# A fused attention, Fourier-mixing and gated-conv kernel: the value windows of its local attention loaded in runs of four heads, eight transfers a unit

## The chip, the cores and the metric

The kernel runs on one core of one Trainium2 chip. The metric is device microseconds of one launch, here the median of three runs. The profile is that of one further execution; its span runs from its first to its last instruction.

## What is computed

Three stages for a batch of 4, sequence length 576, 8 heads of 64 (512 features). All inputs are fp32.

```
x  = pooled attention (q, k, v averaged over groups of 4 tokens, output repeated 4 times)
   + local attention  (mask: |i - j| < 4)
u  = x + real(fft(fft(x, axis=seq), axis=features))
y  = u + relu(layernorm(u) @ w_ch1) @ w_ch2          (512 -> 2048 -> 512)
out = (sigmoid(causal_conv5(y)) * (y @ w_val)) @ w_out
```

Both attentions are `softmax(q k^T / 8) v`, with 1e-9 added to the sum of the exponentials.

## The kernel before, in words

The program is written engine by engine, with semaphores. It has five steps: a first one that does the attention and the mixing of batch 0 (and prepares the weights), a loop of three steps, each of which does the MLP, conv and output of one batch and, between their matmuls, the attention and mixing of the next, and a last step with the MLP, conv and output of batch 3.

**Units.** The attention of a batch is cut into 13 units: 8 pooled ones, one for each head, and NT = 5 local ones (t = 0 to 4). A local unit holds four windows of 32 queries each, for all 8 heads: its scores tile is 128 x 304, with rows = 4 windows x 32 queries and columns = 8 heads x 38 keys. A unit goes through these stages, in different iterations of the program's slots:
- scores (L384 lays the mask, L389 adds q k^T, 16 matmuls of 32 x 76: a pair of heads for one window), 
- subtraction of the row maximum (DVE, L878 and L884), exponential (ACT, L665), the division for local units (DVE, L892 to L898), 
- transposition (PE, L417: four of 128 x 76, one for each pair of heads) and its copy to `probT` (ACT, L673),
- AV (L446 adds the pooled result, L452 the local one: 16 matmuls of 32 x 128, again a pair of heads for one window), and the copy to `x` (ACT, L683 to L686).

On PE the order of the first step is, in each slot: transposition of unit u-2, scores of unit u, AV of unit u-2. So the scores of local unit 2 stand ahead of the AV of unit 0. In the loop the scores of local units stand two slots of the MLP apart, at slots 9, 11, 13, 15 and 17, and the AV three slots behind its scores.

**Loads of a local unit.** `ql`, `kl` and `vl` have two buffers each. SP issues all of these loads, in order, from `attend_loads` and `window` (L336 to L350): first q and k of units 0 and 1, then v of units 0 and 1, then for t = 2, 3, 4 the q and k of unit t (after the scores of unit t-2 have been computed) and the v of unit t (after the AV of unit t-2). For q there is one transfer (L343), for k there are two, one for each head of a pair (L345), and for v four (L349):

```
for s in range(2):
    for j in range(2):
        sp.dma_start(vl[i][LK * j:LK * j + LK, 2 * s:2 * s + 2, :, j, :],
                     v_win[b, t, 32 * s:32 * s + LK, :, j:H:2, 0:D]).then_inc(ld_v[i], 16)
```

Each of them moves 38 rows (keys) x 2 windows x 4 heads (every second one) x 64 floats. In `v_win` the last dimension has 65 floats, so each head's 64 floats are a run of 256 bytes of their own: 304 runs in a transfer, 76 KB. In `vl` rows 0 to 37 hold the keys of the even heads and rows 38 to 75 those of the odd heads, each with zeros in the other head's columns; POOL writes these zeros once (L1239).

**Weights in the first step.** From the slot of local unit 2 on, ACT and DVE also split the weights w1 and w2 into two fp16 parts, in 16 chunks: DVE takes the maximum (L981, `weight_max`), ACT scales (L753, `weight_high`), DVE takes the remainder (L1007, `weight_low`), ACT copies back (L758). The second half of them starts after `weight_scale(1)` (L993 to L1001), which DVE reaches after the folds (`fold`, L925 to L941, with POOL's part at L1204). ACT's queue also issues the loads of w1 and w2, 1 MB each (L736, L739).

Of the kernel before, what the change touches and what calls it, by code (L numbers as in the profile page):

```python
# [19 lines left out]
B, H, N, D = 4, 8, 576, 64  # L20
# [9 lines left out]
LQ, LK = 32, 32 + 2 * BAND  # L30
# [10 lines left out]
WCH = KD * F // WCW  # L41
# [9 lines left out]
def fused_kernel(nc, qk_pool, v_pool, qk_win, v_win, w_ch1, w_ch2, w_val, w_out, taps,  # L51
# [10 lines left out]
    with ctx:  # L62
        def sb(name, shape, dt=fp32):
            return ctx.enter_context(nc.sbuf_tensor(name, shape, dt))
# [6 lines left out]
        w2 = sb("w2", [128, KF, DM])  # L71

        w1s, w2s = (w[:].bitcast(f16).rearrange("p k (f t) -> p k f t", t=2) for w in (w1, w2))
        wmax = sb("wmax", [128, 2, WCH])
        wtop = sb("wtop", [128, 2, 2])
        wscale = sb("wscale", [128, 2])
        unscale = sb("unscale", [128, 1])
        wv = sb("wv", [128, KD, DM])
        wo = sb("wo", [128, KD, DM])
        cw = sb("cw", [128, KD, TAPS])  # L80
# [2 lines left out]
        idb_sb = sb("idb_sb", [128, 128], bf16)  # L83
        sdft = sb("sdft", [128, 3, 2, HS])
        fdft = sb("fdft", [128, 5, HE])
        mhalf = sb("mhalf", [128, 2])

        pair_or_spectrum = sb("pair_or_spectrum", [128, 5 * HS])
        pair_or_folded = sb("pair_or_folded", [128, 3 * HD + 3 * (HD - 2)])
# [5 lines left out]
        vd = sb("vd", [GP, 2, H, D + 1])  # L95
        ql = [sb(f"ql{i}", [128, 4, 128]) for i in range(2)]
        kl = [sb(f"kl{i}", [128, 4, 2, 2 * WK]) for i in range(2)]
        vl = [sb(f"vl{i}", [2 * LK, 4, 4, 2, D]) for i in range(2)]
        mx = sb("mx", [128, 2, H])
        rz = sb("rz", [GQ, 2, 2])  # L100
        lz = sb("lz", [128, 2, H])
# [42 lines left out]
        ld_v = [sem("ld_v0"), sem("ld_v1")]  # L144
# [137 lines left out]
        @block.sync  # L282
        def _(sp):
            def load_pair(b, k):

                free = b * 4 + k - 1 if k >= 2 else b * 4
                if later(free):
                    sp.wait_ge(qk_pooled, free)
                    sp.sem_inc(passed, 1)
                if k == 0 and later(b):  # L290
                    sp.wait_ge(spec, 5 * b)
                    sp.sem_inc(passed, 1)
                if k == 1 and later(b):
                    sp.wait_ge(mixed_o, 3 * b)
                    sp.sem_inc(passed, 1)
                sp.dma_start(raw[k % 2][:], qk_pool[b, k]).then_inc(ld_raw[k % 2], 16)

            def load_v(b, k):
                if later(b):
                    if k == 0:  # L300
                        sp.wait_ge(uT_ps, 6 * b)
                    else:
                        sp.wait_ge(step_over, b)
                    sp.sem_inc(passed, 1)
                sp.dma_start(vraw[k], v_pool[b, k]).then_inc(ld_vraw[k], 16)

            def attend_loads(b):
                load_pair(b, 0)
                load_pair(b, 1)
                load_v(b, 0)  # L310
                if not later(b):
                    load_v(b, 1)
                    sp.dma_start(id_sb[:], ident).then_inc(ld_const, 16)
                    sp.dma_start(idb_sb[:], identb).then_inc(ld_const, 16)
                    for r in range(4):
                        c = 32 * (r % 2)
                        sp.dma_start(mask_sb[32 * r:32 * r + 32, :, :], mask[32 * r:32 * r + 32, :, c:c + LK]).then_inc(ld_const, 16)
                    sp.dma_start(cw[:], taps).then_inc(ld_const, 16)
                load_pair(b, 2)
                load_pair(b, 3)  # L320
                if later(b):
                    load_v(b, 1)

                if not later(b):
                    sp.wait_ge(zeroed, 4)
                    sp.sem_inc(passed, 1)
                window(b, 0, "qk")
                window(b, 1, "qk")
                window(b, 0, "v")
                window(b, 1, "v")  # L330
                for i in range(2, NT):
                    window(b, i, "qk")
                    window(b, i, "v")

            def window(b, t, what):

                done = b * NU + UD + t - 1 if t >= 2 else b * NU
                if later(done):
                    sp.wait_ge(scores if what == "qk" else av_done, done)
                    sp.sem_inc(passed, 1)  # L340
                i = t % 2
                if what == "qk":
                    sp.dma_start(ql[i][:], qk_win[b, t, :, :, 0:128]).then_inc(ld_qk[i], 16)  # L343
                    for j in range(2):
                        sp.dma_start(kl[i][D * j:D * j + D, :, j, :], qk_win[b, t, D * j:D * j + D, :, 128:128 + 2 * WK]).then_inc(ld_qk[i], 16)  # L345
                else:
                    for s in range(2):
                        for j in range(2):
                            sp.dma_start(vl[i][LK * j:LK * j + LK, 2 * s:2 * s + 2, :, j, :],  # L349
                                         v_win[b, t, 32 * s:32 * s + LK, :, j:H:2, 0:D]).then_inc(ld_v[i], 16)  # L350


            attend_loads(0)
            with sp.Fori(0, B - 1) as it:
                attend_loads(it + 1)

            sp.wait_ge(st_out[0], (B * 4 + 1) * 16)
            sp.wait_ge(st_out[1], (B * 4 + 1) * 16)
# [3 lines left out]
        def _(pe):  # L362
            mm = nc.tensor.matmul

            def unit_scores(b, u):
                n = b * NU + u

                read = n - 1 if isinstance(b, int) else n
                if later(read):
                    pe.wait_ge(shifted, read)  # L370
                S = banks(b, u)[0]
                if u == 0 and later(b):
                    pe.wait_ge(uT_sb, 6 * b)
                if u < UD:
                    r0 = D * (u % 2)
                    if u % 2 == 0:
                        pe.wait_ge(qk_pooled, b * 4 + u // 2 + 1)
                    qk = qkd[r0:r0 + D, u // 2, :]
                    for t in range(2):
                        last = mm(S[0:GQ, t * G:(t + 1) * G], qk[:, t * GQ:(t + 1) * GQ], qk[:, 2 * GQ:GT], start=True, stop=True)  # L380
                else:
                    t = u - UD
                    pe.wait_ge(ld_qk[t % 2], 48 * (b * (3 - t % 2) + t // 2 + 1))
                    mm(S[:, 0:H * LK], idb_sb[:], mask_sb[:, t:t + 1, :].to_broadcast([128, H, LK]),  # L384
                       start=True, stop=False, skip_group_check=True)
                    for i in range(4):
                        for w in range(4):
                            c = WK * (w // 2) + 32 * (w % 2)
                            last = mm(S[LQ * w:LQ * w + LQ, 2 * LK * i:2 * LK * (i + 1)], ql[t % 2][:, i, LQ * w:LQ * w + LQ],  # L389
                                      kl[t % 2][:, i, :, c:c + LK], start=False, stop=True, skip_group_check=True)  # L390
                last.then_inc(scores, 1)

# [27 lines left out]
            def unit_av(b, u):  # L420
# [10 lines left out]
                if u < UD:  # L431
                    if u == 0:
                        pe.wait_ge(v_pooled, 2 * b + 2)
                    for t in range(2):
                        for k in range(2):
                            last = mm(R[0:GQ, t * (D + 1):(t + 1) * (D + 1)], PT[0:GP, (2 * k + t) * GQ:(2 * k + t + 1) * GQ],  # L436
                                      vd[:, k, u, :], start=k == 0, stop=k == 1)
                else:
                    t = u - UD
                    if t == 0:  # L440
                        pe.wait_ge(normed, UD * (b + 1))
                        if not later(b):
                            pe.wait_ge(spread_made, 2)
                    for tile, lo, r in ([(LOCAL_TILE[t], 0, 128)] if t < 4 else [(2, 0, 2 * LQ), (5, 2 * LQ, 2 * LQ)]):
                        first = 128 * (tile % 3) + (1 if tile < 3 else 0)
                        mm(R[lo:lo + r, :], spread[:, first:first + r], xd[:, tile // 3, :], start=True, stop=False, skip_group_check=True)  # L446
                    if isinstance(b, int):
                        pe.wait_ge(probT_done, n + 1)
                    pe.wait_ge(ld_v[t % 2], 64 * (b * (3 - t % 2) + t // 2 + 1))
                    for i in range(4):  # L450
                        for w in range(4):
                            last = mm(R[LQ * w:LQ * w + LQ, 2 * D * i:2 * D * (i + 1)], PT[0:2 * LK, i * 128 + LQ * w:i * 128 + LQ * w + LQ],  # L452
                                      vl[t % 2][:, w // 2 + 2 * (w % 2), i, :, :], start=False, stop=True, skip_group_check=True)
                last.then_inc(av_done, 1)

            def mlp_up(b, s):
# [882 lines left out]
```

## Time and profile before

| | us |
|---|---|
| median of 3 runs | 855.63 (854.61 to 857.05) |
| the profiled execution, its own time | 854.21 |
| its span | 852.40 |
| PE busy | 739.1 (87%) |
| DVE busy | 437.0 (51%) |
| ACT busy | 204.5 (24%) |
| POOL busy | 61.2 (7%) |
| DMA packets | 58746, of which 27504 are under 512 B |

Engines: PE is TensorE's matmuls, PEld its weight loads, DVE VectorE, ACT ScalarE, POOL GpSimd, SP SyncE. SPq and ACTq are the issuing of transfers by SyncE and ScalarE. The first step takes from 0 to about 167 us, each of the three steps of the loop about 184 us, the last step the rest. The table's shares are means over all of these.

### The profile page before, as it was taken

Reading aid. Unit: us, or ns where it says so; the run is one execution under the profiler, and the core shown is the slowest. Engines: PE = TensorE matmul, PEld = TensorE weight load, DVE = VectorE, ACT = ScalarE, POOL = GpSimd, SP = SyncE. Lnnn points to the kernel's source line nnn. Section 1 sums busy time; section 2 is a strip of 40 time slices with the busy share of each in tenths; the row PEclk is TensorE's granted clock in tenths of the full one; section 3 lists DMA queues with packets and bytes.
Section 4 is the critical chain, followed back from the end, with each engine's and each line's share of the span. In section 5 each row is a group of like instructions: output and inputs, shape, how many; then the busy total and the mean of one; then the engine's idle time right before and its main releaser. Section 6 shows DMA issues by size and latency. Waiting matters only on the chain.

```text
span 852.4 us, 15400 instructions
## 1 busy us (share of the span) xinstructions
PE 739.1 (87%) x5956; PEld 547.4 (64%) x5956; DVE 437.0 (51%) x955; ACT 204.5 (24%) x409; POOL 61.2 (7%) x80
## 2 busy tenths in 40 slices
PE   1843554689989999899999999899999999999998
PEld 1721222457767677678767667677676777777776
DVE  7832466975445358464354477554263483112542
ACT  1211358512221111222221212122221122111101
POOL 2000021300011021000010020000110120000000
PEclk9999995589999999999999999999999999999999
DMA  9813323260130010441220001711300000000001
GB/s 289 242 47 92 90 71 126 56 152 16 40 83 4 1 57 29 142 77 32 49 49 2 29 29 47 180 26 31 82 13 1 1 28 29 1 2 1 1 12 45
DMA packets 58746, 49.05 MB, mean 58 GB/s; under 512 B 27504, under 2 KB 52208, under 8 KB 57584
## 3 DMA queue, kind: packets, MB, share of 16 engines
q1 hardware_dynamic: 50032, 31.59, 15.0%
q10 hardware_dynamic: 8640, 16.43, 5.6%
q8 instruction: 52, 0.85, 0.4%
q14 instruction: 22, 0.18, 0.1%
HBM read 43.29 MB, written 4.72 MB: 56 GB/s over the span
## 4 chain that ended last, share of the span: by engine, by line
PE 63%; SPq 15%; DVE 9%; issue 5%; DMA 5%; ACT 2%; POOL 1%; DVEq 0%; ACTq 0%; POOLq 0%
PE P L465 19%; PE Y L481 17%; SPq L349 10%; PE P L588 4%; PE Y L588 4%; PE Y L577 4%; PE A L490 3%; SPq L343 3%; DMA kl<-qk_win 2%; SPq L345 2%; PE A L436 2%; PE A L380 2%; PE A L538 1%; PE A L532 1%; DMA vl<-v_win 1%
## 5 line engine op out<-in xcount | busy, mean ns | idle before, releaser
L465 PE MATMUL P<-unT,w 128*128 128x288 f16 x1536 | 215.6, 292 | 8.1 <-issue 4.6
L481 PE MATMUL Y<-hT,w 128*128 128x288 f16 x1536 | 214.9, 286 | 1.5 <-DVE xT L1034 1.5
L1013 DVE SCALAR_TENSOR_TENSOR hT<-P,hT 128x288 f16<-128x288 f32 x128 | 58.4, 457 | 262.2 <-ACT hT L694 262.2
L465 PEld LDWEIGHTS P<-unT,w 128*128 128x128 f16 x1536 | 150.7, 100 | 54.9 <-issue 12.0
L481 PEld LDWEIGHTS Y<-hT,w 128*128 128x128 f16 x1536 | 144.9, 98 | 45.5 <-issue 7.0
L694 ACT ACTIVATE hT<-P 128x288 f16<-128x288 f32 x128 | 52.6, 411 | 198.4 <-PE P L465 198.4
L1049 DVE SCALAR_TENSOR_TENSOR gate<-xT,cw,gate 128x288 f32<-128x288 f32 x128 | 66.4, 519 | 4.5
L665 ACT ACTIVATE prob_or_un<-prob_or_un 73x288 f32<-73x288 f32 (+1 forms) x52 | 23.3, 448 | 171.8 <-DVE prob_or_un L884 171.8
L384 PE MATMUL Y<-mask_sb,idb_sb 128*128 128x304 bf16 x5 | 2.2, 431 | 35.4 <-DMA kl<-qk_win 35.4
L588 PE MATMUL P<-shared,wo 128*128 128x288 f32 x128 | 32.1, 409 | 0.7 <-DVE shared L1061 0.5
L588 PE MATMUL Y<-shared,wo 128*128 128x288 f32 x128 | 32.1, 409 | 0.5 <-DVE shared L1061 0.5
L490 PE MATMUL A<-sdft,pair_or_folded 128*128 128x289 f32 (+5 forms) x102 | 32.4, 442 | 0.0
L577 PE MATMUL P<-xT,wv 128*128 128x288 f32 x128 | 32.2, 406 | 0.0
L577 PE MATMUL Y<-xT,wv 128*128 128x288 f32 x128 | 32.0, 408 | 0.0
L878 DVE TENSOR_REDUCE mx<-A 73x2 f32<-73x288 f32 (+1 forms) x39 | 17.9, 460 | 24.9 <-PE A L389 16.5
L878 DVE TENSOR_REDUCE mx<-Y 73x2 f32<-73x288 f32 (+1 forms) x13 | 5.9, 457 | 47.2 <-PE Y L389 41.7
L588 PEld LDWEIGHTS P<-shared,wo 128*128 128x128 f32 x128 | 24.0, 190 | 8.2 <-DVE shared L1061 1.9
L588 PEld LDWEIGHTS Y<-shared,wo 128*128 128x128 f32 x128 | 24.0, 190 | 7.4 <-DVE shared L1061 1.0
L577 PEld LDWEIGHTS Y<-xT,wv 128*128 128x128 f32 x128 | 24.1, 190 | 6.5
L577 PEld LDWEIGHTS P<-xT,wv 128*128 128x128 f32 x128 | 23.8, 190 | 6.1
L1190 POOL MEMSET x<- 1x512 f32 x4 | 2.1, 517 | 342.6 <-ACT x L683 342.6
L1007 DVE SCALAR_TENSOR_TENSOR w<-w,wscale,gate 128x1024 f16<-128x1024 f32 x16 | 22.9, 1428 | 7.0 <-ACT gate L753 6.9
(141 smaller groups left out, 863.0 us busy)
## 6 DMA issues: line engine op xcount, KB each, us to landing
w<-w_ch ACTq DMA_DIRECT2D x8, 1024.0 KB, 8.7
vl<-v_win SPq DMA_DIRECT2D x80, 76.0 KB
kl<-qk_win SPq DMA_DIRECT2D x40, 140.0 KB, 3.7
ql<-qk_win SPq DMA_DIRECT2D x20, 256.0 KB, 5.1
pair_or_folded<-qk_pool SPq DMA_DIRECT2D x8, 580.0 KB, 5.0
pair_or_spectrum<-qk_pool SPq DMA_DIRECT2D x8, 580.0 KB, 5.5
out<-ot ACTq DMA_DIRECT2D x32, 144.0 KB, 1.8
x<-v_pool SPq DMA_DIRECT2D x4, 576.0 KB
```

The costliest lines, as they stand in the source:

```text
L343: sp.dma_start(ql[i][:], qk_win[b, t, :, :, 0:128]).then_inc(ld_qk[i], 16)
L349: sp.dma_start(vl[i][LK * j:LK * j + LK, 2 * s:2 * s + 2, :, j, :], v_win[b, t, 32 * s:32 * s + LK, :, j:H:2, 0:D]).then_inc(ld_v[i], 16)
L465: last = mm(P[s % 2][:, 0:HN], w1s[:, k, f * 128:(f + 1) * 128, wt], unT[:, ut, k, ha * HN:(ha + 1) * HN], start=k == 0 and wt + ut == 0, ...
L481: last = mm(Y[d][:, 0:HN], w2s[:, f, d * 128:(d + 1) * 128, wt], hT[s % 3][:, ht, :], start=f == 0 and wt + ht == 0, stop=f == KF - 1 and ...
L490: last = mm(bank[0:m, 0:HS], src[0:ROWS[i], i, lo:lo + m], sdft[0:ROWS[i], i, c, :], start=i == 0, stop=i == 2)
L577: last = mm(bank[:, 0:HN], wv[:, k, d * 128:(d + 1) * 128], xT[:, k, TAPS - 1 + ha * HN:TAPS - 1 + (ha + 1) * HN], start=k == 0, stop=k == ...
L588: last = mm(bank[:, 0:HN], wo[:, k, d * 128:(d + 1) * 128], gv[:, k, :], start=k == 0, stop=k == KD - 1)
L665: nc.scalar.activation(p, p, ACT.Exp, scale=(1 / 16 if u < UD else 1) * D ** -0.5).then_inc(exped, 1)
L694: nc.scalar.activation(hT[s % 3][:, 0, :], P[s % 2][:, 0:HN], ACT.Relu).then_inc(hid_hi, 1)
L878: nc.vector.tensor_reduce(mx[0:r, u % 2, 0:g], S, axis=AX.X, op=ALU.max).then_inc(row_max, 1)
L1013: nc.vector.scalar_tensor_tensor(out=hT[s % 3][:, 1, :], in0=P[s % 2][:, 0:HN], scalar=0.0, in1=hT[s % 3][:, 0, :], op0=ALU.max, op1=ALU.s ...
L1049: nc.vector.scalar_tensor_tensor(out=g, in0=xs, scalar=cw[:, d, k:k + 1], in1=g, op0=ALU.mult, op1=ALU.add).then_inc(tap_done, 1)
```

## The change

Slot (i, j) of the score columns (i = 0 to 3, j = 0 or 1) held head 2i + j; now it holds head i + 4j. So PE writes the scores of a pair of heads into two runs of 38 columns that are 76 apart, where it wrote 76 columns in one piece; the transposition is unchanged; and AV writes its 128 columns as two runs of 64 that are 256 apart. `vl` gets the layout (window, j, head, 65), so the four heads of a half are one run of 4 x 65 floats = 1040 bytes in DRAM and in the tile. The four v transfers of 38 rows become eight: for each half j and each pair of windows s one of 32 rows and one of 6. All small tiles of the weights' scaling and `mhalf` become parts of one tile, `small`, which makes room for the larger `vl`.

```diff
-        vl = [sb(f"vl{i}", [2 * LK, 4, 4, 2, D]) for i in range(2)]
+        vl = [sb(f"vl{i}", [2 * LK, 4, 2, H // 2, D + 1]) for i in range(2)]
...
-                    for s in range(2):
-                        for j in range(2):
-                            sp.dma_start(vl[i][LK * j:LK * j + LK, 2 * s:2 * s + 2, :, j, :],
-                                         v_win[b, t, 32 * s:32 * s + LK, :, j:H:2, 0:D]).then_inc(ld_v[i], 16)
+                    for j in range(2):
+                        for lo, rows in ((0, LQ), (LQ, LK - LQ)):
+                            for s in range(2):
+                                sp.dma_start(vl[i][LK * j + lo:LK * j + lo + rows, 2 * s:2 * s + 2, j].rearrange("r w h d -> r w (h d)"),
+                                             v_win[b, t, LQ * s + lo:LQ * s + lo + rows, :, H // 2 * j:H // 2 * j + H // 2, :]
+                                             .rearrange("r w h d -> r w (h d)")).then_inc(ld_v[i], 16)
...
+                    S4 = S[:, 0:H * LK].rearrange("p (i j c) -> p j i c", i=H // 2, j=2)
                     for i in range(4):
+                        half, first = 2 * i // (H // 2), 2 * i % (H // 2)
                         for w in range(4):
                             c = WK * (w // 2) + 32 * (w % 2)
-                            last = mm(S[LQ * w:LQ * w + LQ, 2 * LK * i:2 * LK * (i + 1)], ql[t % 2][:, i, LQ * w:LQ * w + LQ],
+                            last = mm(S4[LQ * w:LQ * w + LQ, half, first:first + 2, :], ql[t % 2][:, i, LQ * w:LQ * w + LQ],
                                       kl[t % 2][:, i, :, c:c + LK], start=False, stop=True, skip_group_check=True)
...
-                    pe.wait_ge(ld_v[t % 2], 64 * (b * (3 - t % 2) + t // 2 + 1))
+                    pe.wait_ge(ld_v[t % 2], 128 * (b * (3 - t % 2) + t // 2 + 1))
                     for i in range(4):
                         for w in range(4):
-                            last = mm(R[LQ * w:LQ * w + LQ, 2 * D * i:2 * D * (i + 1)], PT[0:2 * LK, i * 128 + LQ * w:i * 128 + LQ * w + LQ],
-                                      vl[t % 2][:, w // 2 + 2 * (w % 2), i, :, :], start=False, stop=True, skip_group_check=True)
+                            last = mm(R[LQ * w:LQ * w + LQ, :].rearrange("p (j i d) -> p j i d", j=2, i=4)[:, :, i], PT[0:2 * LK, i * 128 + LQ * w:i * 128 + LQ * w + LQ],
+                                      vl[t % 2][:, w // 2 + 2 * (w % 2), :, i, 0:D], start=False, stop=True, skip_group_check=True)
```

On SP, in the first step, from the q and k of local unit 1 to the v of unit 2 (ql, kl, vl are the tiles written, the numbers are rows x runs x floats of one transfer; `-` is before, `+` is now):

```order
 L343 DMA ql1<-qk_win 128x4x128
 L345 DMA kl1<-qk_win 64x4x140 x2
-L349 DMA vl0<-v_win 38x8x64 x4
-L349 DMA vl1<-v_win 38x8x64 x4
+L350 DMA vl0<-v_win 32x2x260 x2
+L350 DMA vl0<-v_win 6x2x260 x2
+L350 DMA vl0<-v_win 32x2x260 x2
+L350 DMA vl0<-v_win 6x2x260 x2
```

The same four rows follow for `vl1`. Nothing else is moved: where 8 v transfers stood between two q loads, 16 stand now, and where 4 stood, 8 stand.

In the loop each transfer of SP also has an instruction ahead of it that works out its address (ISA); of the v loads of a unit, before (-) and now (+):

```order
-L349 ISA
-L349 DMA vl<-v_win 38x8x64
-L349 ISA
-L349 DMA vl<-v_win 38x8x64
+L350 ISA
+L350 DMA vl<-v_win 32x2x260
+L350 ISA
+L350 DMA vl<-v_win 32x2x260
+L350 DMA vl<-v_win 6x2x260
+L350 ISA
+L350 DMA vl<-v_win 6x2x260
```

Six of the eight transfers of a unit have such an instruction, where all four had one.

## Rows read from the trace of the kernel before

**Rows 1.** The page: the chain that ended last, its shares by engine
```profile
PE 63%; SPq 15%; DVE 9%; issue 5%; DMA 5%; ACT 2%; POOL 1%; DVEq 0%; ACTq 0%; POOLq 0%
```
**Rows 2.** Waits of PE over the span: us in total, times, longest us
```profile
PE Y L384 <- DMA kl<-qk_win: 35.4, 3, 12.6
...
PE P L452 <- DMA vl<-v_win: 9.4, 1, 9.4
...
PE A L384 <- DMA kl<-qk_win: 5.9, 6, 1.3
```
**Rows 3.** Timeline of SP, first step: start us, us, queue, line, transfer
```profile
3.40 2.67 SPq L317 DMA_DIRECT2D mask_sb<-mask  x4
...
9.80 0.62 SPq L343 DMA_DIRECT2D ql<-qk_win  x1
...
12.27 4.21 SPq L343 DMA_DIRECT2D ql<-qk_win  x1
16.52 5.89 SPq L345 DMA_DIRECT2D kl<-qk_win  x2
22.46 28.52 SPq L349 DMA_DIRECT2D vl<-v_win  x8
51.10 2.00 SPq L343 DMA_DIRECT2D ql<-qk_win  x1
...
63.06 6.69 SPq L349 DMA_DIRECT2D vl<-v_win  x4
```
**Rows 4.** Timeline of PE, first step, transposition of unit 0, scores of units 2 and 3, AV
```profile
46.19 1.07 PE L417 MATMUL Y<-id_sb,prob_or_un 128*76 128x128 f32 x4 [0.84 <-DVE prob_or_un L898]
...
57.48 0.41 PE L384 MATMUL Y<-mask_sb,idb_sb 128*128 128x304 bf16 x1 [10.22 <-DMA kl<-qk_win]
...
61.00 1.94 PE L452 MATMUL P<-vl,probT 76*32 76x128 f32 x32
...
76.52 0.41 PE L384 MATMUL Y<-mask_sb,idb_sb 128*128 128x304 bf16 x1 [12.58 <-DMA kl<-qk_win]
```
**Rows 5.** Chain of waits in order of time, 40 to 57 us: start us, us, what
```profile
40.33 2.10 SPq L349
...
53.82 3.52 DMA kl<-qk_win
```
**Rows 6.** Busy time by stretch: us, PE, PEld, DVE, ACT, POOL, granted clock, DMA share, GB/s
```profile
40.00:51.00 11.00, 5.48 (x57) 4.15 (x57) 6.87 (x24) 2.09 (x6) 0.38 (x1) 1.00 0.16 37
51.00:56.00 5.00, 0.00 (x0) 0.00 (x0) 0.00 (x0) 0.00 (x0) 0.00 (x0) 1.00 0.47 113
```
**Rows 7.** All issues of L349: ns min/median/max; from issue to landing of k
```profile
L349 SPq DMA_DIRECT2D vl<-v_win x80: 660/1930/10489, 22.5 to 619.3; - x80
...
DMA to landing us min/median/max: 3.1/3.7/15.8
```
**Rows 8.** First step, timeline of PE, DVE and POOL; DVE busy in one stretch
```profile
95.55 0.41 PE L384 MATMUL Y<-mask_sb,idb_sb 128*128 128x304 bf16 x1 [12.58 <-DMA kl<-qk_win]
...
105.64:132.11 26.47, 18.55 (x43) 0.98 0.31 99
...
112.45 0.42 DVE L928 TENSOR_TENSOR fa<-fa 128x255 f32<-128x255 f32 x1 [6.13 <-POOL fa L1204]
...
111.17 1.25 POOL L1204 TENSOR_TENSOR fa<-x 128x512 f32<-128x512 f32 x1 [6.85 <-issue]
```
**Rows 9.** Loop's first pass, timeline: PE, scores of units 1 to 3; SP, v and q
```profile
219.32 0.30 PE L384 MATMUL A<-mask_sb,idb_sb 128*128 128x304 bf16 x1
...
228.53 0.30 PE L384 MATMUL A<-mask_sb,idb_sb 128*128 128x304 bf16 x1
...
238.93 0.30 PE L384 MATMUL A<-mask_sb,idb_sb 128*128 128x304 bf16 x1 [1.04 <-DMA kl<-qk_win]
...
225.17 7.27 SPq L349 DMA_DIRECT2D vl<-v_win  x4
232.76 1.80 SPq L343 DMA_DIRECT2D ql<-qk_win  x1
```

More of the change, by code:

```diff
@@ L73, in fused_kernel @@
         w1s, w2s = (w[:].bitcast(f16).rearrange("p k (f t) -> p k f t", t=2) for w in (w1, w2))
[L74 to L77, printed above, removed]
+        small = sb("small", [128, 2 * WCH + 4 + 2 + 1 + 2])
+        wmax = small[:, 0:2 * WCH].rearrange("p (i c) -> p i c", i=2)
+        wtop = small[:, 2 * WCH:2 * WCH + 4].rearrange("p (k i) -> p k i", k=2)
+        wscale, unscale = small[:, 2 * WCH + 4:2 * WCH + 6], small[:, 2 * WCH + 6:2 * WCH + 7]
+        mhalf = small[:, 2 * WCH + 7:2 * WCH + 9]
         wv = sb("wv", [128, KD, DM])
@@ L85, in fused_kernel @@
         fdft = sb("fdft", [128, 5, HE])
-        mhalf = sb("mhalf", [128, 2])
         pair_or_spectrum = sb("pair_or_spectrum", [128, 5 * HS])
```

## The prediction

> **What bounds the kernel now.** I read the chain of waits first, then the waits of PE, then the timelines of the engines that these name. The chain that ended last runs 63% through PE but 15% through SP's issuing of transfers [rows 1]: a queue that computes nothing holds about 128 us of the chain. PE itself waits for a transfer of this change's kind in three places [rows 2]: 35.4 us for the keys of the local units in the first step (three waits, so units 2, 3 and 4), 9.4 us once for values (unit 4's AV), and 5.9 us for keys in the loop (six waits, two in each pass). For v itself PE waits once. What it mostly waits for are q and k that stand behind v in SP's queue.
>
> SP's timeline shows how [rows 3]. The eight v transfers of units 0 and 1 hold SP for 28.5 us, 22.46 to 50.98; only then does it issue q of unit 2, whose keys land at 53.82 + 3.52 = 57.34 [rows 5], and PE starts the scores of unit 2 at 57.48 after 10.22 us of idleness [rows 4]. From there it is a cycle: scores of unit t, AV of unit t-2 (ends 62.94 [rows 4]), v of unit t issued (63.06, 6.69 us), q (2.00 us), k, landing, scores of unit t+1 at 76.52. A cycle takes 76.52 - 57.48 = 19.0 us, 5.46 of them on PE and 13.58 on SP and the transfers. Units 3 and 4 both wait so.
>
> **Why a v transfer costs 2.1 us of SP.** Once the weights' traffic is gone, each takes 2.10 us [rows 5], but the shortest of the 80 took 0.66 [rows 7]. So the price of issuing is at most 0.66, and the rest is a queue that drains slowly. While SP issues nothing but v, the 16 DMA engines are busy to 0.16, or 2.6 of them, and move 37 GB/s; when q and k follow, it is 0.47 and 113 GB/s [rows 6]. So 38-row transfers seem to run on two or three engines, and everything behind them queues there: q takes 2.00 us behind v and 0.62 in front of it [rows 3].
>
> The rows alone don't say what a 32-row transfer does. If the eight went at the same 37 GB/s, then 304 runs x 1040 bytes = 316 KB would still need 8.5 us a unit, and nothing would be won. By the Trainium skill ("DMA: Bandwidth & Descriptors", why a DMA increments its semaphore by 16) the number of engines is the largest up to 16 that divides the slowest dimension: 2 for 38 rows, 16 for 32, 6 for 6. By that rule the backlog vanishes, by the row alone the sum would be zero. That 0.16 is close to 2 of 16 engines bears the rule out, so far as this trace can. I forecast with the spread.
>
> **The price of an issue now.** The bounds are 0.33 and 0.75 us: from below an estimate, half of the 0.66 for 304 runs [rows 7], since a transfer now has 64 or 12; from above the mask's four loads, also of 32 rows, at 2.67 / 4 = 0.67 [rows 3], plus some room. I take 0.45, and 0.05 between two, the gap that the 2.10 us rows leave in between: 8 x 0.50 = 4.0 us a unit.
>
> **Sum, part by part** (against the profiled execution's own 854.21 us)
>
> 1. *Scores of unit 2.* SP must finish 16 v issues that begin at 22.46. Alone they would take 8 us. But the first three v transfers take SP from 22.46 to 40.33, 6 us each where the later ones take 2.10 [rows 3, 5]: until about 40 us the loads of w1 and w2 compete. There q, 512 runs, took 4.21 us and k, 512 runs, 5.89 [rows 3], so k's is 11.5 ns a run; v of two units is now 608 runs, or 7 us. Both lie well before 43 us, the latest that would let q and k (1.3 us of issue, 2.8 of landing) be there when PE is ready. PE is ready after the transposition of unit 0, at 46.19 + 1.07 = 47.26, which waits for DVE and not for a load [rows 4]. So unit 2 moves from 57.48 to 47.3: **-10.2**.
> 2. *Two cycles.* v 6.69 to 4.0: -2.7. q behind an empty queue 2.00 to 0.62: -1.4. Landing of k 3.52 to 2.8, an estimate a little below the shortest of 3.1, which was itself behind v [rows 7]: -0.7. That is -4.8 a cycle, a cycle of 14.2 us: **-9.6**. Unit 4's scores thus start at 75.7 where they were at 95.55 [rows 8].
> 3. *What comes due next.* After unit 4's scores DVE is the bound: from 105.64, ten microseconds behind these scores, it does the folds and the rest of the weights until the scale of w2 is ready at 132.11. In these 26.47 us it is busy for 18.55 [rows 8]. So moving unit 4's AV, which waits 9.4 us for its v [rows 2], is worth little by itself: this wait ends beside DVE's work. The largest idle piece of DVE, 6.13, waits for POOL's add, which started 6.85 us late with nothing that the profile shows before it ("issue"), while v and a weight load were in flight [rows 8]. I don't know that it is a matter of transfers. Between 0 and 6.1 I take half: **-3.0**. After the scale of w2 the split weights run through ACT and DVE one chunk after the other and no transfer sets their pace, so the gain is carried to the first matmuls of the MLP.
> 4. *Loop.* The scores of units 1 and 2 are 9.2 us apart, those of 2 and 3, with a wait, 10.4 [rows 9]: a wait costs 1.2. SP's path there is v 7.27, q 1.80 and then k. With two instructions more and six addresses to work out, 8 x (0.45 + 0.18) = 5.0 for v and 0.6 for q make it 3.5 us shorter, against a wait of 1.2. So all six waits go, idle 5.9 us [rows 2] and with PE's restart behind each some 1.0 more: **-6.9**. Even at 0.75 us an issue v takes 7.4, q's 1.2 saved remains, and the waits nearly vanish.
> 5. *At nothing:* the memset of `vl` is 32 floats wider, beside 9 us in which SP has not reached the windows; the two-run writes of PE have no row of their own. From below nothing (as many columns, as many matmuls); the upper bound is with the rivals.
>
> Sum: -10.2 - 9.6 - 3.0 - 6.9 = -29.7, so 824.5 for a profiled execution. The median of before is 1.4 above its profiled execution: **825.9 us**.
>
> **Rivals.**
> - *A, the transfers themselves were the wait.* q and k land no sooner (3.5 stays, q's 2.00 stays), an issue is 0.75, the 16 issues beside the weights finish late, and POOL's pause stays. Then unit 2 gains some 5, each cycle 6.69 - 6.4 = 0.3, the loop 5: 11 in all, about 844. For it speaks that q and k of a unit are 1024 runs, three times v's; against it, that q alone took 0.62 in front of v.
> - *B, no more engines.* The drain stays at 37 GB/s; 8.5 us a unit as before: 855.6, no change. Against it is how different 0.16 and 0.47 are [rows 6].
> - *C, slower: each transfer has a fixed price.* If the 2.10 us were paid for a transfer and not for its runs, eight would hold SP for 17.2 us a unit: in the first step 16.8 later for unit 2 and 8.6 more in each of two cycles and for unit 4's AV, in the loop 8 less a small slack at two places in three passes, some 45. Together +85 or more, 940. It decides above (8.6 + 1.4) / 8 = 1.2 us an issue, where the cycle is as long as now. Against it: the four mask transfers took 2.67 us together, and one v transfer 0.66. The Trainium skill (same page, anatomy of one DMA) gives a DMA of the gpsimd path a fixed 2 us, most of it completion. If these came one after the other here, the result would be this rival. By the mask's row such times overlap.
> - *D, slower: PE pays for broken rows.* If an AV matmul with its output in two runs took twice as long, 1.94 us for a unit [rows 4] would be added to 20 units, 38.8 us (less in the loop, where PE's matmuls are faster): at most 865. Nothing in the trace speaks for it; it decides at about 1.5 us a unit.
> - *E, better.* The pause of POOL goes wholly, issues cost 0.33, and PE, with shorter pauses, does the first step's units at the rate of the loop, where the same mask matmul takes 0.30 and not 0.41 [rows 4, 9]; with some 2 us a cycle more, 812 to 816.
>
> **How the numbers follow.** The forecast 0.68, A 0.12, B 0.06, C 0.04, D 0.03, E 0.07. The forecast's own ends: with 0.33 an issue (1.0 a cycle) and the pause gone (3.1) 821; with 0.75 (2.4 a cycle), unit 2 three later, the pause staying (3.0) and the loop giving 5, 838. The range of 8 in 10 is 816 to 838. Changes under 0.3% (2.6 us) can't be told from none. Faster: forecast, A and E, 0.87; same: B, 0.06; slower: C and D, 0.07.
>
> **What would show it.** In the profile of the changed kernel SP's v issues should have a median under 0.7 us, q's issues in the first step none of 2.0; PE's waits for kl in the first step should be at most 8 us each (zero for unit 2) and none in the loop; unit 2's scores near 47 us, unit 4's near 76, and the scale of w2 between 102 and 112. Wrong would be: v issues above 1.2 us (C, B), or unit 4's scores near 76 with a total above 838, which would mean that something behind DVE's chain was the bound.

## The result, and the profile after

| | us |
|---|---|
| before, median of 4 runs beside it | 855.12 (853.79 to 857.05) |
| after, median of 4 runs | 831.11 (828.80 to 832.66) |
| ratio, 95% interval | 0.972 (0.9701 to 0.9739) |
| profiled execution after: its own time, its span | 832.66, 830.9 |
| PE, DVE, ACT, POOL busy | 740.8, 436.9, 204.6, 61.7 |
| DMA packets, of them under 512 B | 42106, 4784 |

The kernel is 24.0 us faster where 29.2 were forecast. All engines are busy for as long as before, so the whole difference is waiting. The profiled execution of after is the slowest of its four, so the terms below are read against its span: 852.40 - 830.9 = 21.5 us, of one execution of each kernel.

The chain of waits by engine, of after (answers to [rows 1]):

```profile
PE 71%; DVE 12%; issue 6%; SPq 4%; DMA 3%; ACT 2%; POOL 1%; DVEq 0%; POOLq 0%; ACTq 0%
```

SP's issuing has gone from 15% of the span to 4%, PE from 63% to 71%. PE's waits for loads, of after (answers to [rows 2]):

```profile
PE Y L386 <- DMA kl<-qk_win: 19.6, 2, 9.8
...
PE P L456 <- DMA vl<-v_win: 0.4, 1, 0.4
PE A L386 <- DMA kl<-qk_win: 0.3, 1, 0.3
```

Of 35.4 us in the first step 19.6 are left, in two waits and not in three. The waits for v (9.4) and for keys in the loop (5.9) are gone but for 0.4 and 0.3. The timeline of SP in the first step, of after (answers to [rows 3]):

```profile
23.03 11.63 SPq L350 DMA_DIRECT2D vl<-v_win  x16
40.54 0.60 SPq L343 DMA_DIRECT2D ql<-qk_win  x1
...
53.27 5.74 SPq L350 DMA_DIRECT2D vl<-v_win  x8
59.13 0.59 SPq L343 DMA_DIRECT2D ql<-qk_win  x1
```

Sixteen v issues take 11.6 us where eight took 28.5, q behind v takes 0.59 and not 2.00. But the eight of a unit take 5.74 us, where 6.69 were needed for four. The chain of waits in order of time shows the single issues and the landing of k:

```profile
53.27 0.61 SPq L350
53.92 0.60 SPq L350
54.56 0.77 SPq L350
55.37 0.74 SPq L350
...
60.44 3.31 DMA kl<-qk_win
```

By the order of the program the first two are of 32 rows and the next two of 6. The smaller transfers take longer to issue, 0.75 against 0.60, and k lands 3.3 us behind its issue, hardly sooner than before (3.52, [rows 5]). PE's timeline in the first step, scores of units 2, 3 and 4, of after (answers to [rows 4]):

```profile
47.64 0.46 PE L386 MATMUL Y<-mask_sb,idb_sb 128*128 128x304 bf16 x1
...
63.88 0.41 PE L386 MATMUL Y<-mask_sb,idb_sb 128*128 128x304 bf16 x1 [9.74 <-DMA kl<-qk_win]
...
67.40 1.94 PE L456 MATMUL P<-vl,probT 76*32 76x128 f32 x32
...
80.16 0.41 PE L386 MATMUL Y<-mask_sb,idb_sb 128*128 128x304 bf16 x1 [9.81 <-DMA kl<-qk_win]
```

Unit 2 starts 9.8 us earlier and without a wait. The cycle is now 16.3 us, where it was 19.0. An AV still takes 1.94 us, so the writes in two runs cost PE nothing. Behind unit 4's scores, POOL's first add and DVE's wait for it, and the end of the scale of w2, of after (answer to [rows 8]):

```profile
96.06 1.25 POOL L1208 TENSOR_TENSOR fa<-x 128x512 f32<-128x512 f32 x1 [7.13 <-issue]
...
97.34 0.42 DVE L932 TENSOR_TENSOR fa<-fa 128x255 f32<-128x255 f32 x1 [6.38 <-POOL fa L1208]
...
115.48 0.15 DVE L1005 TENSOR_SCALAR small<-small 128x1 f32<-128x1 f32 x1
```

The pause of POOL is still there, 7.13 us. The scale is ready at 115.48 + 0.15 = 115.63, 16.5 us earlier. The loop's first pass, scores of units 2, 3 and 4, of after (answers to [rows 9]):

```profile
213.01 0.30 PE L386 MATMUL A<-mask_sb,idb_sb 128*128 128x304 bf16 x1
...
222.23 0.29 PE L386 MATMUL A<-mask_sb,idb_sb 128*128 128x304 bf16 x1
...
231.89 0.30 PE L386 MATMUL A<-mask_sb,idb_sb 128*128 128x304 bf16 x1 [0.29 <-DMA kl<-qk_win]
```

They are 9.22 and 9.66 us apart, where units 2 and 3 were 10.40 apart [rows 9]. So the 21.5 us are 16.5 in the first step and 5.0 behind it, in the loop.

### The profile page after: what moved, and what is told of

Its sections match the earlier page's. It is cut to its first block, busy times and chain, and to the rows that moved or that the text cites. A ratio compares the mean times of both kernels' runs of the same rounds, so it can differ in the third digit from the quotient of the medians.

```text
span 830.9 us, 15570 instructions
## 1 busy us (share of the span) xinstructions
PE 740.8 (89%) x5956; PEld 548.3 (66%) x5956; DVE 436.9 (53%) x955; ACT 204.6 (25%) x409; POOL 61.7 (7%) x80
## 2 busy tenths in 40 slices
DMA packets 42106, 49.15 MB, mean 59 GB/s; under 512 B 4784, under 2 KB 35568, under 8 KB 40944
## 4 chain that ended last, share of the span: by engine, by line
PE 71%; DVE 12%; issue 6%; SPq 4%; DMA 3%; ACT 2%; POOL 1%; DVEq 0%; POOLq 0%; ACTq 0%
PE P L469 21%; PE Y L485 19%; PE P L592 4%; PE Y L592 4%; PE Y L581 4%; PE A L494 3%; SPq L350 3%; PE A L382 2%; PE A L456 2%; PE A L440 2%; PE A L450 1%; DVE small L985 1%; PE A L542 1%; DMA kl<-qk_win 1%; PE A L536 1%
## 5 line engine op out<-in xcount | busy, mean ns | idle before, releaser
L882 DVE TENSOR_REDUCE mx<-A 73x2 f32<-73x288 f32 (+1 forms) x39 | 18.0, 461 | 20.0 <-PE A L393 10.4
L494 PEld LDWEIGHTS A<-sdft,pair_or_folded 128*128 128x128 f32 (+5 forms) x102 | 15.8, 179 | 17.7 <-issue 8.2
L1011 DVE SCALAR_TENSOR_TENSOR w<-w,small,gate 128x1024 f16<-128x1024 f32 x16 | 22.9, 1428 | 7.0 <-ACT gate L757 6.9
L1194 POOL MEMSET x<- 1x512 f32 x4 | 2.1, 516 | 324.9 <-ACT x L687 324.9
L762 ACT COPY w<-gate 128x1024 f16<-128x1024 f16 x16 | 21.6, 1347 | 8.3 <-DVE w L1011 8.3
```

Source lines behind the costliest of these rows:

```text
L494: last = mm(bank[0:m, 0:HS], src[0:ROWS[i], i, lo:lo + m], sdft[0:ROWS[i], i, c, :], start=i == 0, stop=i == 2)
L762: nc.scalar.copy(wchunk(c, 0), wtmp[:, c % 2, :]).then_inc(w_split, 1)
L1011: nc.vector.scalar_tensor_tensor(out=wchunk(c, 1), in0=wchunk(c), scalar=wscale[:, i:i + 1], in1=wtmp[:, c % 2, :], op0=ALU.mult, op1=ALU. ...
```

## The experiments

Two questions were open. What did the change win by, the long runs, the split into 32 and 6 rows, or both? And what holds the time that was forecast to go and didn't: the order of SP's queue, the price of an issue, POOL's pause? Nine kernels were run, each timed in three rounds beside the kernel before on the same chip. Kernels that were timed beside different runs of before are compared by their ratio to it, or the difference by the ratios stands in brackets behind that of the medians.

### Long runs with 38 rows

```diff
-                        for lo, rows in ((0, LQ), (LQ, LK - LQ)):
+                        for lo, rows in ((0, LK),):
...
-                    pe.wait_ge(ld_v[t % 2], 128 * (b * (3 - t % 2) + t // 2 + 1))
+                    pe.wait_ge(ld_v[t % 2], 64 * (b * (3 - t % 2) + t // 2 + 1))
```

> The changed kernel with its layout and its 1040-byte runs, but four v transfers of 38 rows in place of eight of 32 or 6. Theory 'spread' (38 rows run on few DMA engines, 32 rows on many, and that is what the change won): a v issue stays near 2.1 us where nothing competes, the DMA share while only v is issued stays near 0.16, a cycle of the first step stays near 19 us (unit 4's scores near 95), total 850 to 856. Theory 'run length' (four times fewer runs is what it won): an issue falls to 0.8 us or less, a cycle is 5.5 on PE plus 3.0 for v, 1.9 for q and k and 3.3 of landing, 13.7 us, unit 4's scores near 75, total near 827.

Measured: 842.32 us, ratio 0.9869 (0.9844 to 0.9893). It lies between the two theories. From its chain of waits in order of time:

```profile
59.21 0.66 SPq L350
...
62.12 0.93 SPq L343
...
64.46 6.74 DMA kl<-qk_win
```

A v issue takes 0.66 us, so theory 'spread' is wrong on it. But k lands 6.74 us behind its issue, against 3.31 in the changed kernel. So SP is held less, four issues of 2.80 us in all, while the transfers behind v are held more. Unit 3's scores start at 71.33 and unit 4's at 88.69, a cycle of 17.4 us. The queue's backlog has left SP, where a row shows it, for the time from issue to landing. Long runs alone give 11 of the 24 us. In the profiled executions 5.3 of its 13.9 us come up to the first matmul of the MLP (161.9 against 167.2) and 8.6 behind it, where PE has no wait for keys at all. In the first step a part of the gain is lost again on POOL, whose pause is longer here than anywhere else:

```profile
107.22 1.26 POOL L1208 TENSOR_TENSOR fa<-x 128x512 f32<-128x512 f32 x1 [9.76 <-issue]
```

Where SP is held shows in the chain of waits of the kernel before, at the v of unit 2, whose four transfers have short runs:

```profile
63.06 0.66 SPq L349
63.76 1.72 SPq L349
65.52 2.09 SPq L349
67.65 2.10 SPq L349
```

The first one, with nothing of v in front of it, takes 0.66 us, as the long runs do; only those behind it take more. So 0.66 is the price of the issue itself, for 304 runs as for 76, and the rest is waiting for the queue.

### The split with short runs

```diff
-                    for s in range(2):
-                        for j in range(2):
-                            sp.dma_start(vl[i][LK * j:LK * j + LK, 2 * s:2 * s + 2, :, j, :],
-                                         v_win[b, t, 32 * s:32 * s + LK, :, j:H:2, 0:D]).then_inc(ld_v[i], 16)
+                    for j in range(2):
+                        for lo, rows in ((0, LQ), (LQ, LK - LQ)):
+                            for s in range(2):
+                                sp.dma_start(vl[i][LK * j + lo:LK * j + lo + rows, 2 * s:2 * s + 2, :, j, :],
+                                             v_win[b, t, LQ * s + lo:LQ * s + lo + rows, :, j:H:2, 0:D]).then_inc(ld_v[i], 16)
```

This is against the kernel before, whose heads keep their order; PE waits for 128 in place of 64.

> The kernel before with its layout and its 256-byte runs, but each v transfer of 38 rows split into one of 32 and one of 6. Theory 'spread': an issue takes 0.6 to 0.8 us, a cycle about 16.3 us as in the changed kernel, total 829 to 833. Theory 'run length': the queue drains 1216 runs a unit as before, 8.4 us, plus four more issues; a cycle of 19 us or more, total 855 or above.

Measured: 830.50 us, ratio 0.9717 (0.9685 to 0.9749). The changed kernel's is 0.972. SP and PE in its timeline:

```profile
52.66 5.75 SPq L350 DMA_DIRECT2D vl<-v_win  x8
...
79.35 0.41 PE L385 MATMUL Y<-mask_sb,idb_sb 128*128 128x304 bf16 x1 [9.69 <-DMA kl<-qk_win]
```

Eight issues of 5.75 us, a cycle of 16.2: the whole gain, with runs of 256 bytes and with the heads where they were. The pairing of heads i and i + 4, the new layout and the longer runs add nothing that can be measured once the rows are split.

### 19 and 19 rows

```diff
-                        for lo, rows in ((0, LQ), (LQ, LK - LQ)):
+                        for lo, rows in ((0, LK // 2), (LK // 2, LK // 2)):
```

> The changed kernel with its 38 rows cut into 19 and 19 in place of 32 and 6: again eight transfers a unit, the same runs, the same bytes. Theory 'divisor' (the number of DMA engines is the largest up to 16 that divides the rows: 2 for 38, 1 for 19): all of v runs on one engine; at half of the 37 GB/s that 38 rows had, 316 KB need 17 us a unit, the DMA share while v alone runs is near 0.06, k lands more than 10 us after its issue, a cycle of the first step is 23 us or more and the total is above 860. Rival 'any short transfer spreads': issues of 0.6 to 0.75 us, a cycle of 16.3, total 831.

Measured: 913.72 us, ratio 1.0708 (1.0686 to 1.0731). The rival, 831, is refuted. Waits of PE and a stretch in which SP issues v and nothing else:

```profile
PE Y L386 <- DMA kl<-qk_win: 53.7, 3, 19.4
PE A L386 <- DMA kl<-qk_win: 28.0, 6, 5.4
PE P L456 <- DMA vl<-v_win: 14.0, 1, 14.0
```

```profile
73.50:81.00 7.50, 0.00 (x0) 0.00 (x0) 0.00 (x0) 0.56 (x1) 0.00 (x0) 1.00 0.06 20
```

The columns are those of [rows 6]. The share of 16 DMA engines is 0.06, that is one engine, at 20 GB/s. With 38 rows it was 0.16 and 37 GB/s in [rows 6]; in the cleaner stretch of the kernel before, in which SP issues the v of unit 2 and nothing else, it is two engines of 16:

```profile
63.10:69.80 6.70, 0.84 (x4) 0.36 (x2) 0.00 (x0) 0.58 (x1) 0.00 (x0) 1.00 0.12 27
```

A cycle of 19 and 19 rows is 23.5 us. So with the same bytes, runs and number of transfers, 32 + 6 rows give 831 us and 19 + 19 give 914. That the rule holds by divisors is the Trainium skill's ("DMA: Bandwidth & Descriptors", why a DMA increments its semaphore by 16): 1 engine for 19 rows, 2 for 38. The traces agree, with 0.06 for 19 and 0.12 for 38, where 1 and 2 of 16 would be 0.0625 and 0.125. That k landed more than 10 us behind its issue was wrong: it was 6.2. By estimate the 316 KB of a unit take 15.8 us at 20 GB/s, and about half of that is waited for while SP still issues (8.4 us for eight). The issues show how the backlog reaches SP; the first four take 0.65, 0.65, 0.61 and 0.61 us, and then:

```profile
75.25 0.96 SPq L350
76.25 1.66 SPq L350
```

### Four transfers a unit

```diff
-                            for s in range(2):
-                                sp.dma_start(vl[i][LK * j + lo:LK * j + lo + rows, 2 * s:2 * s + 2, j].rearrange("r w h d -> r w (h d)"),
-                                             v_win[b, t, LQ * s + lo:LQ * s + lo + rows, :, H // 2 * j:H // 2 * j + H // 2, :]
-                                             .rearrange("r w h d -> r w (h d)")).then_inc(ld_v[i], 16)
+                            sp.dma_start(vl[i][LK * j + lo:LK * j + lo + rows, :, j].rearrange("r w h d -> r w (h d)"),
+                                         v_win[b, t, lo:lo + rows, :, H // 2 * j:H // 2 * j + H // 2, :]
+                                         .rearrange("r w h d -> r w (h d)")).then_inc(ld_v[i], 16)
...
-    v_win = np.ascontiguousarray(np.stack(v_tiles, axis=1))
+    v_win = np.stack(v_tiles, axis=1)
+    v_win = np.ascontiguousarray(np.concatenate([v_win[:, :, 0:LK], v_win[:, :, LQ:LQ + LK]], axis=3))
```

PE waits for 64 in place of 128.

> The changed kernel with its values laid out in DRAM so that the four windows of a unit follow each other (a few rows stand twice): four v transfers of 32 or 6 rows x 4 runs a unit in place of eight of 32 or 6 rows x 2. If an issue has a price of its own (0.60 for 32 rows, 0.75 for 6 rows), v takes 2.8 us of SP in place of 5.7, a cycle of the first step 13.4 in place of 16.3, unit 4's scores are 5.8 us earlier, near 74, and the total is near 825. If the price goes by runs, v stays at 5.7 and the total at 831.

Measured: 825.27 us, ratio 0.9672 (0.9644 to 0.9700). Its timeline of SP, and PE at unit 4's scores:

```profile
52.77 2.85 SPq L349 DMA_DIRECT2D vl<-v_win  x4
...
74.14 0.41 PE L385 MATMUL Y<-mask_sb,idb_sb 128*128 128x304 bf16 x1 [7.03 <-DMA kl<-qk_win]
```

Twice the runs in a transfer, and the issues still take 0.60 and 0.76 us: the price is the transfer's, not the runs'. Unit 4 starts 6.0 us earlier than in the changed kernel, and the median is 5.8 lower (by the ratios, 4.1).

### POOL's pause: an add behind the first all-reduce, and one ahead of it

```diff
                 nc.gpsimd.partition_all_reduce(wtop[:, 1, i:i + 1], wtop[:, 0, i:i + 1], 128,
                                                bass.bass_isa.ReduceOp.max).then_inc(w_all, 1)
+                if i == 0:
+                    pt(warm[:, 0:1], warm[:, 1:2], warm[:, 2:3], ALU.add).then_inc(warmed, 1)
+                    pool.wait_ge(warmed, 1)
+
+            nc.gpsimd.memset(warm[:], 0.0)
```

> The changed kernel with one add of 128 x 1 on POOL right behind its first all-reduce, where POOL is idle. Theory 'first call' (POOL's pause of 7.1 us before its first 128 x 512 add is the loading of code after the all-reduce): the pause moves to the small add, POOL's fold starts right behind its memsets, DVE's wait of 6.4 us in the folds goes, total 5 to 6 us lower, 825 to 826. Theory 'transfers in flight' (the pause comes from loads that go on at that time): the pause stays where it is, total 831.

The second kernel has the same add, without its semaphore, after POOL's setup and ahead of the first step.

> The changed kernel with the small add on POOL ahead of its first all-reduce and not behind it. If the pause belongs to the first add of the program, it is paid early and the total is 825, as in e6. If it is the all-reduce that makes the next other instruction pay, the pause of 7 us before the fold stays and the total is 831.

Measured: behind it 824.33 us, ratio 0.9668 (0.9635 to 0.9701); ahead of it 829.49 us, ratio 0.9748 (0.9707 to 0.9790), with runs from 826.5 to 835.5, too wide to decide by time alone. POOL's timeline, the add behind:

```profile
44.16 0.38 POOL L1239 PARTITION_ALL_REDUCE small<-small  x1 [29.15 <-DVE small L992]
51.59 0.18 POOL L1242 TENSOR_TENSOR warm<-warm 128x1 f32<-128x1 f32 x1 [7.05 <-issue]
...
89.20 1.31 POOL L1210 TENSOR_TENSOR fa<-x 128x512 f32<-128x512 f32 x1
```

And the add ahead:

```profile
14.50 0.19 POOL L1252 TENSOR_TENSOR warm<-warm 128x1 f32<-128x1 f32 x1 [0.32 <-issue]
43.24 0.38 POOL L1238 PARTITION_ALL_REDUCE small<-small  x1 [28.55 <-DVE small L991]
...
94.69 1.25 POOL L1209 TENSOR_TENSOR fa<-x 128x512 f32<-128x512 f32 x1 [6.69 <-issue]
```

An add that comes before the all-reduce pauses for 0.32 us, and it doesn't spare the later one its 6.69. An add behind the all-reduce pauses for 7.05, in a stretch in which the DMA engines are busy to 0.03 and POOL had nothing else to do, and the later one starts at once. So the pause hardly needs transfers in flight; it belongs to the first add behind the first all-reduce. The memsets between the two (L1194 and L1195 in the changed kernel) don't pay it. Its length is another matter: 6.7 to 7.1 us in eight of the kernels, but 7.94 (q and k ahead, on the kernel before), 8.90 (19 rows) and 9.76 (38 rows, long runs) in three of the four whose v goes in 38 or 19 rows. That transfers in flight can lengthen it is likely from this and not shown. Behind the second all-reduce no pause is seen, in any of the kernels; of the changed one:

```profile
114.49 0.38 POOL L1237 PARTITION_ALL_REDUCE small<-small  x1 [8.47 <-DVE small L990]
130.33 0.98 POOL L257 TENSOR_TENSOR x<-x,fb 128x256 f32<-128x256 f32 x1 [15.46 <-DVE fb L956]
```

This add starts 0.18 us behind the result of DVE that it waits for. Whether the pause lay hidden in those 15.46 us or did not occur, the traces don't say. The early add was worth 6.3 us at its place, the end of the scale of w2 moving from 115.6 to 109.3; the medians are 6.8 apart (by the ratios, 4.4). The Trainium skill ("GPSIMD Engine Reference", on dispatch) has a loading of code of about 6 us, with no instruction of its own in the profile, at the first call of a freshly loaded kernel. The 6.7 to 7.1 us are near it, but no run here shows what is loaded.

### q and k ahead of v in the queue

```diff
                 for i in range(2, NT):
                     window(b, i, "qk")
+                for i in range(2, NT):
                     window(b, i, "v")
```

Once with the changed kernel, once with the kernel before.

> The changed kernel with q and k of units 2, 3 and 4 standing ahead of their v in SP's queue. Theory 'the wait is the order' (q and k of the next unit wait in the queue behind a v whose own wait is for an AV): PE's waits for kl in the first step go, 19.6 us; a cycle is PE's own 6.5 us; unit 3's scores near 54, unit 4's near 61 in place of 80; v still lands in time for its AV within 1 us; the scale of w2 stays 35 us behind unit 4's scores, near 96; total near 812. Rival 'DVE becomes the bound' (shift, division, maximum and remainder of 5.5 us a unit, and all of the weights' chunks behind them): unit 4's scores are near 61 all the same, but the scale of w2 comes more than 40 us behind them and the total is 818 or above.

> The kernel before with the same order of the queue and nothing of the change: 38-row transfers of 256-byte runs. If the order is what costs, unit 2's scores stay at 57.5 (16 k's and the eight v of units 0 and 1 stand before them), units 3 and 4 follow at 64 and 71, the waits in the loop go as well, and the total is near 823, below the changed kernel. If the slow drain costs by itself (k behind v on the same engines, v too late for the AV), it is 835 or above.

Measured: with the changed kernel 810.14 us, ratio 0.9505 (0.9468 to 0.9542); with the kernel before 829.15 us, ratio 0.9716 (0.9693 to 0.9739). PE's timeline of the first, scores of units 3 and 4, two AVs, and DVE's end of the scale of w2:

```profile
53.27 0.46 PE L387 MATMUL Y<-mask_sb,idb_sb 128*128 128x304 bf16 x1
...
59.57 0.46 PE L387 MATMUL Y<-mask_sb,idb_sb 128*128 128x304 bf16 x1
...
62.15 1.08 PE L457 MATMUL P<-vl,probT 76*32 76x128 f32 x32
...
72.56 1.93 PE L457 MATMUL P<-vl,probT 76*32 76x128 f32 x32 [2.60 <-DMA vl<-v_win]
```

```profile
94.17 0.15 DVE L1006 TENSOR_SCALAR small<-small 128x1 f32<-128x1 f32 x1
```

No scores wait; a cycle is 6.3 us; unit 4's scores are at 59.6 where they were at 80.2; and the scale is 34.7 us behind them. So DVE doesn't become the bound: the 20 us pass through. v is late by up to 2.6 us for its AV, where 1 was expected, beside DVE's work. And PE itself gets faster: behind a stretch without a wait, an AV takes 1.08 us where all of the kernel before take 1.94 in the first step, with a granted clock of 1.00, the upper of its two levels, in both stretches. The last one, behind its wait and with 0.50 granted, the lower level, takes 1.93 again. The waits of PE, of the second:

```profile
PE P L453 <- DMA vl<-v_win: 18.5, 3, 8.1
...
PE Y L385 <- DMA kl<-qk_win: 10.4, 1, 10.4
```

Here unit 2's scores still wait 10.4 us behind the eight slow v transfers, and v, at its old pace, is late for three AVs. That lies between the two numbers on record: the order takes the waits for k away and a part comes back as waits for v. With nothing but one more loop line, which moves q and k ahead, the kernel before reaches what the change reached.

### All three

The order, the four transfers and the add behind the all-reduce, on the changed kernel.

> The changed kernel with the order of e4, the four v transfers of e3 and the early add on POOL of e6. If the three are independent where they act (the order takes 19, the pause 6, and the four transfers nothing more once nothing waits for them), total 805 to 807. If the pause was partly covered or DVE has no room left, 810 or above.

Measured: 803.07 us (800.90 to 806.37), ratio 0.9406 (0.9383 to 0.9429). That is 50 us less than before, and below the 805 to 807 of its expectation. Against the order alone the median is 7.1 lower, and the scale of w2 is ready 7.5 us earlier (86.8 against 94.3). In the changed kernel the pause was worth 6.3. PE's waits for v, 3.7 us in two with the order alone, are gone too, but they stood beside DVE's work; what the four transfers add can't be told from none.

## Why the prediction was right, and where its sizes were off

The time, 831.11, is in the range (816 to 838) and 5.2 above the forecast of 825.9. Of the profiled executions, 29.7 were forecast and 21.5 came. The way and the cause were forecast; that the time lies so well inside the range owes something to its width of 22 us.

- *The bound* was read rightly: q and k waited in SP's queue behind v. The kernel with only its order changed shows it most directly.
- *Why v costs 2.1 us* was read rightly, too: few engines. 19 rows on one engine give the opposite sign, 32 + 6 with short runs the whole gain. What the rows did not say, and the forecast took from the rule on divisors, the 19 rows have now shown. Rival B, that the number of engines stays, is refuted by the q issue of 0.59 us behind v.
- *Step 1, unit 2's scores*: forecast -10.2, measured -9.8. The sixteen issues took 11.6 us beside the weights, not 7, well before they were needed.
- *Step 2, two cycles*: forecast -9.6, measured -5.5 (80.16 - 47.64 = 32.5 against 95.55 - 57.48 = 38.1). This term was mis-sized most. An issue was taken as 0.45 us; it is 0.60 for 32 rows and 0.75 for 6, so v takes 5.74 and not 4.0. The error was to take runs for the measure and to halve the shortest v issue. The 0.66 were the first issue of each group of four, with nothing of v in front, and q's 0.62 in [rows 3] was for 512 runs: both spoke against a price by runs. The upper row, the mask's 0.67 for 32 rows, was the near one: four transfers with twice the runs show that there is a price of its own. And k's landing stayed at 3.3, where 2.8 had been estimated below the shortest row. Of rival A that much was true.
- *Step 3, what comes due next*: forecast -3.0, measured -1.1. DVE was named rightly as the next bound. The pause of POOL was halved for want of knowledge; it stayed whole. The 1.1 are DVE's second wait for POOL in the folds (1.16 us), which hung on unit 4's AV and has gone.
- *Step 4, loop*: forecast -6.9, measured -5.0; by the distance of the outputs' first matmuls the second and third pass are 2.0 shorter each, and the first 0.9. The waits have gone but for 0.3, so the mechanism is right. The size can't be called wrong: from the first matmul of the MLP to the end it is 685.2 us before and 680.2 after, but 676.1 and 675.4 with POOL's add behind and ahead, whose loop is the same. Single executions differ here by more than the 1.9 in question.
- *Rival C*, a price for each transfer: it exists, at 0.6 to 0.75 us, under the 1.2 at which it would have decided. (That threshold counted 8.6 us for the v of a unit; with the cycle's own 6.69 it is (6.69 + 1.4) / 8 = 1.0.) Seen in this light it costs the change 2.9 us a unit, which the four transfers give back.
- *Rival D*, broken rows: AV 1.94 us before and after, nothing.
- *Rival E*, better: neither the pause nor the price of an issue fell, and PE kept its pace (mask 0.41 us, AV 1.94) in the cycle. Its faster pace did come where the order had taken the waits away, with an AV in 1.08 us.
- *The signs*: four of those named did not come. The median of v's issues over the whole program was 0.74 us, not under 0.7; PE's waits for keys in the first step were 9.7 and 9.8 us, not at most 8; unit 4's scores were at 80.2, not near 76; and the scale of w2 was ready at 115.6, not between 102 and 112. All four follow from the price of an issue and the pause. Unit 2's scores at 47.6 and the gone waits for q came as said.

## What to carry to other kernels

Look at the number of rows of a transfer before its bytes: here 38 rows, cut into 32 and 6, left the two DMA engines that they had run on and took 24 us off the kernel, while 19 and 19 added 60. Then look at what stands in a queue behind a transfer that itself has to wait: the loads that are needed first, q and k, stood behind v, whose own wait was for a later instruction, and this order was worth another 21 us (by the ratios, 18) with no transfer changed. And price an issue by the transfer, about 0.6 to 0.75 us on this queue, not by its runs.

## What the runs showed of the hardware that I had not expected

- A transfer of 6 rows takes longer to issue than one of 32: 0.75 against 0.60 us, in the changed kernel and in those with short runs and with four transfers, whether with 2, 4 or 8 runs a row.
- A backlog can stand in two places. With short runs on 38 rows SP itself is held from the second transfer on (1.72, then 2.10 us an issue, and 0.66 for the first); with 19 rows and long runs from the fifth on (0.96, then 1.66); with long runs on 38 rows SP is free after 0.66, and what is issued next lands late (6.74 against 3.31). Issue times alone would have called it solved.
- The first add on POOL behind the program's first all-reduce begins some 7 us late (7.05, 6.69, 7.13, and up to 9.76 beside v in 38 rows); an add ahead of it doesn't help, and one of 128 x 1 right behind it does. Behind the second all-reduce, where the add waits 15.46 us for DVE, nothing of it is seen.
- PE did the same AV in 1.94 us and in 1.08 us at the same granted clock of 1.00; the shorter time stands behind a stretch in which it had not waited.
